# Two attention, gate and expert layers on one core: another order of the first loads, splits and product steps, and two PSUM bank pairs for the first folded-weight pieces

## The reference, cut to what matters

```python
# q, k, v: 8 x 8 heads x 576 x 64;  p: 8 x 8 x 32 x 64
p_packed = sm_attn(p, k, v)                # softmax attention of 32 packed queries
x = sm_attn(q, p_packed, p_packed)         # then 576 queries on 32 keys
x = x.transpose(0, 2, 1, 3).reshape(4608, 512)
xn = x / rms(x) * rms_g                    # gated layer, 1536 wide
x = (silu(xn @ w_gate) * (xn @ w_val)) @ w_out
h = ((x @ w1) * (x @ w2)) @ w3             # second layer, 1024 wide
out = h @ w_out2
```

## Time and profile before

| | |
|---|---|
| median of 3 runs | 1437.08 us (1435.96 to 1438.87) |
| the profiled execution, own time | 1435.77 us |
| its span | 1434.0 us |
| PE busy in the span | 1407.0 us (98%) |
| DVE busy | 606.9 us (42%) |
| ACT busy | 398.2 us (28%) |
| POOL busy | 140.0 us (10%) |
| mean granted clock of PE | 0.993 of full |

### The profile page before, as it was taken

The page is one execution under the profiler, slowest core; times in us unless marked ns, Lnnn a source line. Parts: engine busy times, 40 slices in busy tenths (PEclk is TensorE's granted clock), DMA queues, the critical chain, the costliest instruction groups (busy, mean ns, idle before and its releaser), DMA issues.

```text
span 1434.0 us, 23119 instructions
## 1 busy us (share of the span) xinstructions
PE 1407.0 (98%) x9952; PEld 1204.8 (84%) x9952; DVE 606.9 (42%) x1119; ACT 398.2 (28%) x787; POOL 140.0 (10%) x137
## 2 busy tenths in 40 slices
PE   6979999999999999999999999999999999999999
PEld 4749889889898898898989988888888888888887
DVE  2646656546556565466565652212122121212111
ACT  2334333332433433324233332111111111111111
POOL 0010100100001001000010230202102020202000
PEclk9989999999999999999999999999999999999999
DMA  7922112021131220210104120101010110100000
GB/s 232 372 73 85 42 58 78 10 86 51 26 88 40 65 71 9 86 51 26 35 26 164 47 76 30 59 1 59 0 59 0 60 57 2 59 1 30 1 30 30
DMA packets 35861, 85.12 MB, mean 59 GB/s; under 512 B 2992, under 2 KB 12208, under 8 KB 34736
## 3 DMA queue, kind: packets, MB, share of 16 engines
q1 hardware_dynamic: 35760, 83.65, 17.5%
HBM read 62.65 MB, written 20.99 MB: 58 GB/s over the span
## 4 chain that ended last, share of the span: by engine, by line
PE 95%; DVE 2%; issue 1%; ACT 1%; DMA 1%; POOL 0%; SPq 0%; POOLq 0%; DVEq 0%
PE psum L564 9%; PE psum L563 9%; PE psum L565 9%; PE psum L528 8%; PE psum L544 7%; PE psum L546 7%; PE psum L529 7%; PE psum L530 7%; PE psum L545 7%; PE psum L584 5%; PE psum L585 5%; PE psum L583 5%; PE psum L494 4%; PE psum L507 1%; PE psum L477 1%
## 5 line engine op out<-in xcount | busy, mean ns | idle before, releaser
L528 PE MATMUL psum<-a_hi,m_hi 128*128 128x288 f32 x768 | 242.9, 316 | 0.5 <-DVE g_s L945 0.2
L529 PE MATMUL psum<-a_lo,m_hi 128*128 128x288 f32 x768 | 227.0, 296 | 0.0
L530 PE MATMUL psum<-a_hi,m_lo 128*128 128x288 f32 x768 | 226.6, 295 | 0.0
L544 PE MATMUL psum<-g_hh,wo_hi 128*128 128x288 f32 x768 | 226.2, 295 | 0.0
L545 PE MATMUL psum<-g_hl,wo_hi 128*128 128x288 f32 x768 | 225.9, 294 | 0.0
L546 PE MATMUL psum<-g_hh,wo_lo 128*128 128x288 f32 x768 | 225.9, 294 | 0.0
L563 PE MATMUL psum<-xh,w_hi 128*128 128x512 f32 x576 | 224.1, 389 | 0.0
L564 PE MATMUL psum<-xl,w_hi 128*128 128x512 f32 x576 | 224.1, 389 | 0.0
L565 PE MATMUL psum<-xh,w_lo 128*128 128x512 f32 x576 | 224.1, 389 | 0.0
L979 DVE TENSOR_TENSOR b_h<-b_s,psum 128x512 f32<-128x512 f32 x72 | 49.5, 688 | 408.6 <-PE psum L565 408.6
L528 PEld LDWEIGHTS psum<-a_hi,m_hi 128*128 128x128 f32 x768 | 144.6, 188 | 57.3 <-issue 52.3
(11 more groups left out here) (105 smaller groups left out, 1701.8 us busy)
## 6 DMA issues: line engine op xcount, KB each, us to landing
kT<-in_kT SPq DMA_DIRECT2D x8, 1152.0 KB, 5.3
v_sb<-in_v SPq DMA_DIRECT2D x16, 576.0 KB, 4.6
qT<-in_qT SPq DMA_DIRECT2D x16, 576.0 KB, 3.8
y_scratch<-g_res SPq DMA_DIRECT2D x16, 576.0 KB, 3.1
x_raw<-y_scratch SPq DMA_DIRECT2D x9, 1024.0 KB, 7.6
out<-b_res SPq DMA_DIRECT2D x8, 1024.0 KB, 5.1
w_raw<-in_w SPq DMA_DIRECT2D x2, 2048.0 KB, 10.5
w_in<-in_w_gate SPq DMA_DIRECT2D x4, 768.0 KB, 9.1
```

The source lines that it names most:

```text
L528: nc.tensor.matmul(in_ps[which], hi, a2_hi[:, t, par, :], start=par == 0, stop=False)
L529: nc.tensor.matmul(in_ps[which], hi, a2_lo[:, t, par, :], start=False, stop=False)
L530: last = nc.tensor.matmul(in_ps[which], lo, a2_hi[:, t, par, :], start=False, stop=par == 1)
L544: nc.tensor.matmul(out_ps[m], hi, hh[:], start=f == 0, stop=False)
```

## The change

In words: SP loads the first chunks of `wout` and `w3a` ahead of `pT` and `kT`, and the others of half 0 ahead of `q(0,0)`. PE runs `fuse(0,0)` ahead of `S1(0,0)`. ACT and DVE split chunks 1, 2 and 3 one item earlier. In half 1, ACT casts chunk 0 ahead of the copy of `PT` and chunk 2 behind `exp2(0,0)`; DVE evicts its two banks of `wf` behind `normalize2(0,0)`. `M(0,1)` and `M(0,3)` write banks 4 and 5, and `M(0,1)` to `M(0,3)` wait for the item before the last one only. `M(0,0)` to `M(0,3)` wait for the DVE part of the first `wf` eviction, and the first `outof` for `M(0,3)` to be read. `wf_second` moves to memory of `wout_lo`; the waits of `g_hh`, `g_hl` and of the first four `wo_split` for `wf_stored` are gone.

```diff
-            wout_hi, wout_raw, wout_lo = split_pair("wout")
+            wout_hi = at("wout_hi", [P, FC2, DM], F32R)
+            with ExitStack() as st2:
+                wout_raw = alloc(st2)("wout_raw", [P, FC2, DM])
+            with ExitStack() as st2:
+                alloc(st2)("wf_pad", [P, 4, DM])
+                wf_second = alloc(st2)("wf_second", [P, 4, DM])
+            wout_lo = at("wout_lo", [P, FC2, DM], F32R)
...
+        def m_bank(a, part):
+            return 4 if a == 0 and part in (1, 3) else 6
...
+            load_fuse(0, 0)
             load_kp(0)
-            load_fuse(0, 0)
+            load_fuse(0, 1)
             load_v(0, 0)
-            load_fuse(0, 1)
+            load_fuse(0, 2)
+            load_fuse(0, 3)
             load_q(0, 0)
             sp.dma_start(gcol[:], g_d).then_inc(g_loaded, 16)
-            load_fuse(0, 2)
-            load_fuse(0, 3)
             load_v(0, 1)
...
                 n = number[kind, a, part]
+                if kind == "M" and a == 0 and 1 <= part <= 3:
+                    n -= 1
                 if n:
                     pe.wait_ge(xy_free, n)
...
                         pe.wait_ge(w_in_loaded, 16 * 2 * KC)
+                        pe.wait_ge(wf_dve, 2)
...
                 pe.wait_ge(hl_ready, n + 1)
+                if n == 0:
+                    freed(pe, "M", 0, 3)
...
             pe.wait_ge(const_ready, 3)
+            fuse(0, 0)
             item("S1", 0, 0)
-            fuse(0, 0)
             fuse(0, 1)
...
             def wo_split(f):
                 act.wait_ge(fuse_done, 2)
-                act.wait_ge(wf_stored, 32)
+                if f >= 4:
+                    act.wait_ge(wf_stored, 32)
...
# ACT
             fuse_split(0, 0)
+            fuse_split(0, 1)
             item("S1", 0, 0)
-            fuse_split(0, 1)
+            fuse_split(0, 2)
             item("AT", 0, 0)
-            fuse_split(0, 2)
+            fuse_split(0, 3)
             item("PV", 0, 0)
-            fuse_split(0, 3)
             fuse_split(0, 4)
...
             fuse_split(0, 7)
+            fuse_split(1, 0)
             item("PT", 0, 0)
-            fuse_split(1, 0)
             fuse_split(1, 1)
             wf_evict(0)
+            exp2(0, 0)
             fuse_split(1, 2)
-            exp2(0, 0)
...
-                        if n == 0:
-                            act.wait_ge(wf_stored, 32)
...
# DVE: the order of the splits as on ACT, the wait at n == 0 gone too, and
             shift2(0, 0)
+            fuse_split(1, 2)
+            item("G", 0, 0)
+            sums2(0, 0)
+            normalize2(0, 0)
             wf_evict(0)
-            item("G", 0, 0)
-            fuse_split(1, 2)
-            sums2(0, 0)
             fuse_split(1, 3)
-            normalize2(0, 0)
```

More of the change, by code:

```diff
@@ L165, in build @@
         g_s, g_h = const("g_s", [P, HALF]), const("g_h", [P, HALF])
-        with ExitStack() as st:
-            wf_second = alloc(st)("wf_second", [P, 4, DM])
         g_hh = [const(f"g_hh{i}", [P, HALF], F32R) for i in range(2)]
@@ L493, in item @@
                             rows, cols = slice(DH * par, DH * (par + 1)), slice(NP * c, NP * (c + 1))
-                            last = nc.tensor.matmul(xy[par][cols, :], ppTg[rows, cols], w_in[rows, c, at:at + BANK],
+                            last = nc.tensor.matmul(psum[cols, m_bank(a, part) + par, :], ppTg[rows, cols], w_in[rows, c, at:at + BANK],
                                                     start=True, stop=True)
@@ L660, in item @@
                     at = FF * which + BANK * group
-                    nc.scalar.copy(m_hi[:, :, at:at + BANK], psum[:, 6:8, :]).then_inc(m_hi_ready, 1)
+                    bank = m_bank(a, part)
+                    nc.scalar.copy(m_hi[:, :, at:at + BANK], psum[:, bank:bank + 2, :]).then_inc(m_hi_ready, 1)
             def exp2(a, t):
@@ L820, in item @@
                     at = FF * which + BANK * group
-                    nc.vector.tensor_tensor(m_lo[:, :, at:at + BANK], psum[:, 6:8, :], m_hi[:, :, at:at + BANK].bitcast(F32),
+                    bank = m_bank(a, part)
+                    nc.vector.tensor_tensor(m_lo[:, :, at:at + BANK], psum[:, bank:bank + 2, :], m_hi[:, :, at:at + BANK].bitcast(F32),
                                             ALU.subtract).then_inc(xy_free, 1)
@@ L959, in _ @@
                         dve.wait_ge(hh_ready, n + 1)
-                        if n == 0:
-                            dve.wait_ge(wf_stored, 32)
                         nc.vector.tensor_tensor(g_hl[f % 2][:], g_h[:], g_hh[f % 2][:].bitcast(F32), ALU.subtract).then_inc(hl_ready, 1)
```

## The result

The changed kernel takes 1419.80 us (median of 4 runs, 1419.32 to 1421.0), against 1436.52 (4 runs, 1435.69 to 1438.87) before: ratio 0.9882, 95% interval 0.9865 to 0.9899. That is 16.7 us, or 1.2%, faster. The profiled execution is the slowest of the four, 1421.0 us with a span of 1418.9; its span is 15.1 us under the old one.

A forecast was written before the change was run, and what follows sets the result against it. Only PE's waits and low clock in the first 100 us could be saved, as PE is full afterwards. -10.45 + 2.8 (queue) + 1.7 (clock) - 7.0 (M) = -12.95; against 1437.08 this gave 1424.1 us, range 1416.5 to 1430.5.

The forecast's parts named there:

- rival (a): At `S2(0,1)`: the transfer queue does not hold PE up, so no stall; 1419.6 us, chance 0.17.
- Part 1: Start to `S1(0,1)`: with `fuse(0,0)` first and earlier splits, PE's waits and low clock go; 10.45 us earlier.
- Part 2, the queue: At `S2(0,1)`: PE stalls 3.0 us for `q(0,1)`, landing at 49.3 in a saturated batch; +2.8 us in the sum.
- The clock: Behind the stall at `S2(0,1)`: PE drops to half speed for a stretch, costing 1.7 us (bounds 0 and 2.5).
- part 3: From `M(0,0)` to the first `g_s`: two bank pairs for M save 7.0 us (8.2 at full speed, 6.3 at half).
- The r trip: Store of `rr` and its way back, queued behind `wo_raw`, ahead of `m_hi(0)`; a wait there was a sign of error, unpriced.
- T3: Theory formed on the trace after: the r trip behind `wo_raw` sets the head's end; removing the `qT` wait alone gains nothing.
- Rival (b): The M pieces gain little, 0 to 2 us, because ACT and DVE serve them no faster; 1430 us, chance 0.07.
- At nothing: `wf_second`, dropped `wf_stored` waits, DVE's later `wf_evict(0)` and chunk (1,2) cast behind `exp2(0,0)`: priced at no effect.

The follow-up runs named there:

- the run without the edits costed at nothing: Changed kernel with the `wf_stored` waits back and the half 1 orders of ACT and DVE as before: 1419.53 us.
- the mark: The changed kernel itself, unaltered, run again beside its neighbours on the same chip: 1419.81 us.
- both moves: Changed kernel with `q(0,1)` loaded ahead of the second quarter of `w_in`, and the r trip ahead of two loads of `wo_raw`: 1418.85 us.

## Why the prediction was right, and where its sum was off

The direction and the mechanism hold; the forecast of 1424.1 was 4.3 us too high, inside the range, and the time is that of rival (a), whose mechanism did not occur; that its number fits is luck. Of the 4.3 us, 1.8 are the sum's: between the two profiled executions lie 14.8 us (1435.77 to 1421.0), where the sum had 12.95. The other 2.5 are the distance of these executions from their medians, 1.3 before and 1.2 after. Step by step:

**Part 1**, -10.45: PE was ready for `S2(0,1)` at 45.94 (45.71 + 0.23) instead of 56.8, -10.86. The start at 7.85 came out to the digit. The low clock at the start lasted about 3.3 us (the last of the 0.43 us steps begins at 10.55), not 5.1. The two experiments that undo the loads and the splits (4.4 and 10.5 slower) show both parts at work; they are not shares of the gain.

**Part 2, the queue**, +2.8: the step is "I take 49.3". `q(0,1)` was issued at 39.87 and landed 7.8 us later, at 47.7. The batch took 26.5 us from the issue of `v(0,1)`, not 27.7: `v(0,1)` itself 4.7 instead of 5.7, and 347 GB/s over the stretch instead of 316. (The batch's own 8.26 MB in 26.5 us are 312 GB/s, and 289 before; 347 and 316 count all that moved, so they include what was issued behind `q(0,1)`. Rival (a) divided the batch's bytes by such a rate and so came out too early.) So the stall was 1.7, not 3.0, and rival (a), no stall, did not occur. Without the stall `M(0,0)` would have come only about 0.4 us earlier, as DVE was next in line; the prediction took the head behind `S2(0,1)` to move with PE and did not look at DVE's order there. By the Trainium skill, DMA: Bandwidth & Descriptors, Where 436 GB/s comes from, loads from HBM run at about 358 GB/s, and the prediction's estimate from it was 46.6, 1.1 us too early. The 347 of this stretch are near that figure, but no limit is to be read from it here: from 4 to 8 us of the changed kernel, with loads alone, 416 GB/s were moved.

**The clock**, +1.7, and **part 3**, -7.0: these are the terms that were mis-sized. In one execution the clock held behind the `qT` wait and fell ahead of `M(0,2)` (0 and -5.7: from `M(0,0)` to `g_s` 11.4 us instead of 17.1); in the other it fell behind `qT` and held in `M` (+1.6 and -8.4, 8.6 us). I charged the drop in full behind `qT` and once more, in part, by taking 7.0 of 8.2 in `M`. The two terms are tied by the r trip: an `M(0,0)` that comes 1.8 us later finds it nearly done, and `M(0,2)` starts only 0.4 later (76.63 against 76.20). That the clock falls at one of the two places and not at the other is no rule: in the run without the edits costed at nothing it held at both (waits of 1.52 and 2.38), with one bank pair it fell at both. The sums come to -15.0 and -15.9, and the spans to -15.1 and -16.1.

**The r trip** is the wait that I had named as a sign of error and not priced. The store of `rr` waited behind `wo_raw`, and `M(0,2)` came 4.9 us after `M(0,0)` instead of 3.8: 1.1 us, and the clock with it. Its place in the queue matters most where the loads ahead of it are late: added to the early `q(0,1)` the move of the trip brought 4.1 us on the same chip (1422.92 to 1418.85), alone 0.6. So T3 holds for `M(0,2)`, but for the wait for `qT` it is not the first cause: DVE's order takes all but 0.4 us of it ahead of `M(0,0)` already.

**Rival (b)** fell by two runs (8.1 and 8.7 us). The Trainium skill, TensorE: Matmul & The Clock Gate, HAM oscillation, has no further gain from double-buffered PSUM in its kernel (there once the loop had been reordered so that PE stayed busy); no run here is of that kind. Here each piece waited 2.4 us for its own eviction, and the pairs are about half of the gain. **At nothing** held, within 0.3 us, in the changed kernel; that DVE's new place for `wf_evict(0)` costs about 1.3 us where `q(0,1)` is early is argued from the profiles, not run.

**The signs.** Named and seen: the start at 7.9, no gap over 0.3 us up to `S2(0,1)`, a wait there, PE full from 85 us. Missed: that wait was 1.7 us (2 to 4 named), `M(0,0)` to the first `g_s` took 11.4 and 8.6 us (9 to 11 named), and the clock fell behind `qT` in one profile of two.

What stays open: the time of the changed kernel between its two courses was seen in two profiled executions only, so how often each occurs is not known. The loss of 3.1 us with an early `q(0,1)` is one of medians; between the profiled executions of that run and of the mark it is 2.5 us, and so much later is `g_s` (84.23 against 81.75).

## What to carry to other kernels

When a stage is shortened, ask of each transfer in it what releases its issue: what PE itself releases moves with PE, but in a saturated queue it still lands only when all ahead of it has. A tiny round trip behind megabytes of loads with later deadlines is a candidate for pulling ahead (4.1 us where these loads were late, nothing clear otherwise), but its way back then shares the queue with them; a load pulled ahead of others is not, if SP then stands at its wait while the queue runs dry. And in a turn of matmul, cast and difference over one PSUM pair, each piece costs the sum of the three; a second pair that lies free for that stage brought this from 4.4 us a piece to 3.5 to 4.9 for two. Before a wait is priced at its length, look at what the next engine has in its own order at that place: here DVE took 1.3 of the 1.7 us.

## What the runs showed of the hardware

The length of a gap does not decide alone whether PE's clock falls. After waits of 1.69 and 1.79 us at the same place, the granted clock stayed at 1.00 in one execution and was 0.64 over the next 4 us in another, of the same kernel. Ahead of `M(0,2)` it stayed after 1.57 us in all five profiles that have this gap, and after 2.10, 2.16 and 2.38 in three other kernels, while it fell after 1.84 (the two pairs alone), 2.0 (both moves, 0.64 in 76 to 80 us), 2.95 (the changed kernel, 0.57 there) and 5.24 (early `q(0,1)`). The same gap of 2.27 us ahead of the fourth `fuse` step was followed by 0.50 in the kernel before and by 1.00 in two others. Half speed was worth 1.6 us each of the three times that it came behind `qT`: 25.1 us from `S2(0,1)` to `M(0,0)` instead of 23.5.

A small store behind a backlog lands with the backlog. 2.2 KB took 4.1 us in the changed kernel and 2.2 when sent 1.8 us later, landing at the same time to 0.1 us; it took 5.7 where the loads ahead were late, and 1.4 with two of the three loads put behind it.
